# A fused attention and two-stage expert kernel: tails first in the last pair, a branch and the last y moved, first weights loaded behind a transfer

## What is computed

```python
scores = q @ k.T / 8
scores = where(scores >= max(scores) - tau, scores, -1e9)
attn = softmax(scores);  x = (attn @ v)         # heads side by side: 2304 x 512
logits = normed(x) @ normed(expert_emb).T / moe_tau
e = argmax(logits);  gate = softmax(logits)[e]
x = gate * (relu(x @ w1[e]) @ w2[e])            # w1: 512 x 1024, w2: 1024 x 512
h = x @ w_in;  g = max(h, 0) + alpha * min(h, 0)
out = g @ w_out                                 # w_in: 512 x 2048, w_out: 2048 x 512
```

## Time and profile before

| | us |
|---|---|
| median of 3 runs | 1055.79 (1053.36 to 1055.9) |
| the profiled execution | 1049.71 |
| its span, first to last instruction | 1048.0 |
| PE busy in the span | 1018.3 (97%) |
| granted TensorE clock, mean | 0.991 |
| PE busy in 30 to 40 us | 6.82 of 10 |
| PE busy in 60 to 120 us | 59.75 of 60 |
| PE busy in 345 to 375 us | 22.28 of 30 |
| PE busy in 375 to 623 us | 248.00 of 248 |
| PE busy in 623 to 640 us | 14.32 of 17 |
| DVE, ACT, POOL busy in the span | 528.6, 391.0, 336.3 |

### The profile page before, as it was taken

How to read it: one execution, slowest core, us unless ns; L and a number is a source line. 1 busy time by engine, 2 the same in 40 slices (tenths; PEclk the granted TensorE clock), 3 DMA queues, 4 the chain that set the end, 5 groups by cost and what they waited for, 6 DMA issues and landing times.

```text
span 1048.0 us, 19527 instructions
## 1 busy us (share of the span) xinstructions
PE 1018.3 (97%) x6559; PEld 893.6 (85%) x6560; DVE 528.6 (50%) x1203; ACT 391.0 (37%) x814; POOL 336.3 (32%) x443
## 2 busy tenths in 40 slices
PE   8899999999999699999999999999999999999997
PEld 7788898898898578888888878999999899999996
DVE  5778887987987312222221326644444444444442
ACT  5677676776776032222222323221111121111211
POOL 2233334312113596799776361010010010100101
PEclk9999999999999799999999999999999999999999
DMA  5765767767562655465535245000000000000000
GB/s 157 174 140 121 196 168 190 173 161 216 122 143 87 218 191 187 136 199 196 204 127 198 99 164 169 31 25 9 29 31 31 1 30 30 30 0 0 31 1 30
DMA packets 103502, 116.36 MB, mean 111 GB/s; under 512 B 70268, under 2 KB 70300, under 8 KB 102916
## 3 DMA queue, kind: packets, MB, share of 16 engines
q1 hardware_dynamic: 88228, 87.51, 30.2%
q10 hardware_dynamic: 11056, 13.69, 4.1%
q0 software_dynamic: 4144, 14.20, 3.8%
HBM read 68.53 MB, written 18.82 MB: 83 GB/s over the span
## 4 chain that ended last, share of the span: by engine, by line
PE 85%; DMA 4%; DVE 4%; SPq 4%; issue 1%; ACT 1%; POOL 0%; ACTq 0%; POOLq 0%; DVEq 0%
PE bank L682 75%; PE bank L685 9%; DMA k_st<-k_both 3%; SPq L435 1%; SPq L446 1%; DVE probs L1301 1%; DVE neg_max L1293 1%; DVE q_lo L1318 0%; DMA y_sorted<-x_sorted 0%; DMA x_sorted<-X,pos 0%; ACT q_hi L1083 0%; DMA x_row<-x_sorted 0%; SPq L414 0%; SPq L453 0%; SPq L474 0%
## 5 line engine op out<-in xcount | busy, mean ns | idle before, releaser
L682 PE MATMUL bank<-x_hi,ring 128*128 128x384 f32 x768 | 210.8, 337 | 1.3 <-DVE act L1648 1.3
L682 PE MATMUL bank<-ring,g_hi 128*128 128x512 f32 x576 | 179.1, 392 | 0.0
L1235 ACT ACTIVATE g_hi<-act 128x384 fp32r<-128x384 f32 x96 | 50.4, 525 | 303.3 <-DVE act L1648 300.9
L585 POOL TENSOR_TENSOR ring<-stage,ring 128x2048 fp32r<-128x2048 f32 x32 | 147.1, 4598 | 4.8
L682 PEld LDWEIGHTS bank<-x_hi,ring 128*128 128x128 f32 x768 | 140.3, 188 | 5.0 <-DVE act L1648 1.6
L1645 DVE TENSOR_SCALAR neg<-bank,alpha_col 128x384 f32<-128x384 f32 x96 | 59.2, 617 | 144.0 <-PE bank L682 144.0
L682 PE MATMUL bank<-x_lo,ring 128*128 128x384 f32 x384 | 128.9, 336 | 0.0
L1293 DVE TENSOR_REDUCE neg_max<-bank 128x1 f32<-128x576 f32 x144 | 104.3, 753 | 38.0 <-PE bank L682 37.0
L682 PEld LDWEIGHTS bank<-ring,g_hi 128*128 128x128 f32 x576 | 106.8, 188 | 18.7 <-DVE g_lo L1596 0.3
L1067 ACT ACTIVATE probs<-bank,neg_max 128x576 f32<-128x576 f32 x144 | 103.1, 740 | 48.9 <-DVE neg_max L1293 48.8
L682 PE MATMUL bank<-k_st,q_st 128*128 128x288 f32 (+5 forms) x696 | 114.7, 306 | 3.7 <-DVE probs L1301 3.4
(11 more groups left out here) (183 smaller groups left out, 1416.7 us busy)
## 6 DMA issues: line engine op xcount, KB each, us to landing
stage<-in_moe_w SPq DMA_DIRECT2D x32, 1024.0 KB, 5.5
k_st<-k_both SPq DMA_DIRECT2D x60, 288.0 KB
x_row<-x_sorted ACTq DMA_DIRECT2D x23, 296.0 KB, 2.9
y_sorted<-y_row ACTq DMA_DIRECT2D x21, 256.5 KB, 2.6
q_st<-q_hi SPq DMA_DIRECT2D x30, 160.0 KB
q_st<-q_lo SPq DMA_DIRECT2D x30, 160.0 KB
qraw<-in_q SPq DMA_DIRECT2D x16, 256.0 KB, 3.2
vraw<-in_v SPq DMA_DIRECT2D x16, 256.0 KB, 4.9
```

Of the source, the lines that this page charges most:

```text
L585: nc.gpsimd.tensor_tensor(lo, src, hi.bitcast(F32), ALU.subtract).then_inc(piece_lo, 2)
L682: return nc.tensor.matmul(dst, lhsT, rhs, start=start, stop=stop)
L1235: nc.scalar.activation(g_hi[f % 3][:, :], act2[f % 2][:, :], ACT.Copy).then_inc(g_hi_ready, 1)
```

## The change

Five things. (1) In the last pair the tail unit is processed first, so its rows are stored earlier; X's tiles are numbered anew (tail tiles 12 and 13), group 3 is tiles 13 to 15 and group 4 tiles 16 and 17, and DVE and PE weave these two groups into the last units. SP stores both tail halves; ACT did one of them before. (2) `WARM` goes from 26 to 34, and 7 more such matmuls follow `turn_slot(0)`. (3) On PE a slot is cut in two (`slot_first`, `slot_last`), so that the loop's branch comes between `second_first` and `turn_slot` rather than at the slot's end, the last slot's `slot_last` stands behind the loop, and one more expert number is read in each slot. `EARLY` is one lower. (4) In the last stage the last y is copied and stored inside the first blocks, and the pieces of the second matrix start with one rather than two. (5) Expert 0's first weights are no longer loaded at the start: the first 1 MB follows pair 1's spreads and v, the second follows pair 3's spreads.

```diff
-EARLY = MIN_SLOTS - 2
+EARLY = MIN_SLOTS - 3
-WARM = 26
+WARM, WARM_SPLIT = 34, 7
-ROUTES = ((0, 4), (4, 4), (8, 5), (13, 4), (17, 1))
-TAIL_TILES = (12, 17)
+ROUTES = ((0, 4), (4, 4), (8, 5), (13, 3), (16, 2))
+TAIL_TILES = (12, 13)
+        def unit_at(n, j):
+            return (j + UNITS - 1) % UNITS if n == PAIRS - 1 else j
@@ SP
             load_k(sp, 2, 0)
-            load_pieces(sp, 0, 0)
-            load_pieces(sp, 0, 2)
...
-                    if n in (4, 6, 8, 10):
-                        sp.wait_ge(piece_lo, n - 2)
+                    if n in (2, 4, 6, 8, 10):
+                        if n > 2:
+                            sp.wait_ge(piece_lo, n - 2)
                         load_pieces(sp, *((0, n) if n < PIECES else (1, n - PIECES)))
                     if n:
                         sp.wait_ge(pv_done, UNITS * n)
                     load_v(n + 1, 1 - par)
+                    if n == 0:
+                        load_pieces(sp, 0, 0)
...
-            sp.wait_ge(x_ready, UNITS * PAIRS)
-            store_tail(sp, PAIRS - 1, (0,))
+            sp.wait_ge(x_ready, UNITS * (PAIRS - 1) + 1)
+            store_tail(sp, PAIRS - 1, (0, 1))
@@ PE, behind the last pair
             turn_out(last_pair, UNITS - 2)
+            rank(3)
             turn_out(last_pair, UNITS - 1)
-            rank(3)
             rank(4)
@@ PE, slots
+            def slot(i, more):
+                if not static(i):
+                    slot_last(i - 1, None if static(i, 1) else half_of(i - 2))
+                slot_first(i)
...
-            for_slots(pe, slot)
+            for_slots(pe, slot, load_last)
+            last_slot, e_last, half_last, half_before_last = late
+            slot_last(last_slot, half_before_last)
@@ ACT, last stage
-                    if static(g) and f < PIECES - 2:
-                        late_hi_parts(2 + f, 3 + f)
+                    if static(g) and f < PIECES - 1:
+                        late_hi_parts(f + 1, f + 2)
+                    if static(g) and f == 1:
+                        store_y(last_slot)
...
-            late_hi_parts(0, 2)
-            store_y(last_slot)
+            late_hi_parts(0, 1)
@@ DVE, behind the last pair
             normalise(PAIRS - 1, UNITS - 3)
-            normalise(PAIRS - 1, UNITS - 2)
-            normalise(PAIRS - 1, UNITS - 1)
             for k in range(7):
                 route_step(3, k)
+            normalise(PAIRS - 1, UNITS - 2)
             route_step(3, 10)
             for k in (7, 8, 9):
                 route_step(3, k)
+            normalise(PAIRS - 1, UNITS - 1)
@@ DVE, last stage
-            copy_y(last_slot, LAST_BANK)
...
+                    if static(g) and f == 0:
+                        late_lo_parts(0, 1)
                     low(g, f)
-                    if static(g) and f < PIECES - 2:
-                        late_lo_parts(2 + f, 3 + f)
+                    if static(g) and f == 0:
+                        copy_y(last_slot, LAST_BANK)
+                    if static(g) and 0 < f < PIECES:
+                        late_lo_parts(f, f + 1)
-            late_lo_parts(0, 2)
+            dve.wait_ge(late_hi, 1)
```

More of the change, by code:

```diff
@@ L303, in build, with is_tail, heads_of, short @@
         o_stored = [sem(f"o_stored{i}") for i in range(GT)]
+        def unit_at(n, j):
+            return (j + UNITS - 1) % UNITS if n == PAIRS - 1 else j
+        def is_tail(n, j):
+            return unit_at(n, j) == MAIN
+        def heads_of(n, j):
+            return (0,) if is_tail(n, j) else (0, 1)
+        def short(n, j):
+            return 1 if n == PAIRS - 1 and j else 0
         def tile_no(n, j, h=0):
-            return TILES_PAIR * n + 2 * j + h
+            return TILES_PAIR * n + 2 * j + h - short(n, j)
         def turn_no(n, j, w):
-            return TURNS_PAIR * n + (3 * j + w if j < MAIN else 3 * MAIN + (1 if w else 0))
+            return TURNS_PAIR * n + 3 * j - short(n, j) + (w if not is_tail(n, j) else 1 if w else 0)
+        def last_main(n, j):
+            m, i = before(n, j)
+            return last_main(m, i) if is_tail(m, i) else (m, i)
         def before(n, j):
@@ L339, in group_of, with for_slots @@
             return (m, g) if g >= 0 and m < PAIRS else None
-        def for_slots(eng, body):
+        def for_slots(eng, body, between=None):
             end = eng.value_load(slot_end[0:1, EXPERTS - 1:EXPERTS], min_val=MIN_SLOTS + 1, max_val=SLOTS + 1)
@@ L346, in for_slots @@
             body(1, True)
+            if between:
+                between()
             with eng.Fori(2, EARLY) as i:
@@ L606, in small_steps @@
                 for j in range(UNITS):
-                    for h in heads_of(j):
+                    for h in heads_of(n, j):
                         pool.wait_ge(max_ready, tile_no(n, j, h) + 1)
@@ L728, in scores @@
                 if not (static(n) and j == 0):
-                    last_no = tile_no(n, j - 1, h) if j else (tile_no(n - 1, MAIN) if h == 0 else tile_no(n - 1, MAIN - 1, 1))
+                    last_no = tile_no(*last_main(n, j), 1) if h else tile_no(*before(n, j))
                     pe.wait_ge(probs_ready, last_no + 1)
@@ L736, in scores @@
                     jobs = []
-                    for x in (heads_of(0) if j == MAIN else (h,)):
+                    for x in ((0, 1) if u == MAIN else (h,)):
                         for part in range(2):
@@ L747, in scores @@
                     for i, (x, to, keys) in enumerate(jobs):
-                        last = mm(to, q_st[par][:, x, j * P:(j + 1) * P], keys, i == 0, i == len(jobs) - 1)
+                        last = mm(to, q_st[par][:, x, u * P:(u + 1) * P], keys, i == 0, i == len(jobs) - 1)
                 last.then_inc(scores_ready, 1)
@@ L784, in values @@
                 tail = probsT[buf][:, 2 * MAIN * P:2 * SEQ]
-                if j < MAIN:
+                if not is_tail(n, j):
                     for c in range(CHUNKS):
@@ L843, in pair @@
                         scores(*nxt, 0)
-                    if more and nxt[3] < MAIN:
+                    if more and not is_tail(nxt[0], nxt[3]):
                         scores(*nxt, 1)
@@ L886, in _, with warm_up @@
             turn_out(last_pair, UNITS - 2)
+            rank(3)
             turn_out(last_pair, UNITS - 1)
-            rank(3)
             rank(4)
             pe.wait_ge(piece_lo, PIECES)
-            for _ in range(WARM):
-                mm(bank[:, M_BANK, :], ring[:, 0, 0:P], ring[:, 0, 0:D], True, True)
+            def warm_up(n):
+                for _ in range(n):
+                    mm(bank[:, M_BANK, :], ring[:, 0, 0:P], ring[:, 0, 0:D], True, True)
+            warm_up(WARM)
             H_BANK, HT_BANK, X_BANK, Y_BANK = (0, 1), (2, 3), 4, 5
@@ L942, in second_first, with half_of, slot_first @@
                 second(half_at, range(FC - 2))
-            def slot(i, more):
+            def half_of(i):
+                return expert_of(i)[1]
+            def slot_first(i):
                 e, half_at = expert_of(i)
@@ L955, in slot, with slot_last @@
                     second_first(i - 1, e_before, half_before)
+            def slot_last(i, half_before, more=True):
                 if more:
@@ L1328, in normalise @@
                 got = bank[:, turn_bank(n, j), TURN_AT:TURN_AT + TURNED]
-                if j < MAIN:
-                    at_x = x_tile(n, j) * XC + n % 4 * TURNED
+                if not is_tail(n, j):
+                    at_x = x_tile(n, unit_at(n, j)) * XC + n % 4 * TURNED
                     V.tensor_tensor(X[:, at_x:at_x + TURNED].rearrange("p (h d) -> p h d", h=2),
```

44 lines of the change are left out of this document (21 added, 23 removed).

## The result

| | before | after |
|---|---|---|
| median of the timed runs, us | 1054.57 (1053.03 to 1055.9, 4 runs) | 1040.21 (1037.66 to 1042.18, 4 runs) |
| ratio | | 0.9863, 95% interval 0.9835 to 0.9891 |
| the profiled execution, us | 1049.71 | 1037.66 |
| its span, us | 1048.0 | 1036.0 |

The changed kernel is 1.4% faster: 14.4 us by the medians (interval 11.5 to 17.4), 12.0 us between the two profiled executions. The direction was right, and PE's idle times at 34 us, behind the slots and ahead of the last stage are gone as forecast; the sizes were too small.

The account below looks back on a forecast made before the run. PE was taken to bound the kernel, full almost everywhere, so only its idle time could go. The terms -2.9 + 0.2 - 2.4 - 2.7 = -7.8 us took the median from 1055.79 to 1048.0 us, range 1044.5 to 1052.5.

Parts of the forecast that it names:

- Term A: Start: with the weights behind pair 1's spreads, these land earlier and PE's 34 us stall goes; -2.9 us, bounds 1.3 and 3.0.
- term B: Last pair, routing and first slots: earlier scatters and a full clock in slot 0; -2.4 us, bounds 1.0 and 3.1.
- term C: Slots to last stage: PE's waits of 1.42 us (branch) and 1.27 us (DVE's first act) go; -2.7 us.
- term A2: Pair 3: the second MB of weights behind its spreads costs a little; +0.2 us, bounds 0 and 1.2.
- was 6.1 below the median; the terms don't depend on that: Sum: the terms of the profiled execution, 1049.71 us, carry over unchanged to the median, from 1055.79 to 1048.0 us.
- 3.0 if all of the stall goes: Start: upper bound of the gain from moving the weights, PE's stall at 34 us being 2.98 us.
- they end 1.0 us after the rows have landed: Before slot 0: the extra matmuls end at 359.6, the rows land at 358.6, so PE turns them 1.4 us earlier.
- One more register load in each slot: Rival, slots: the third load uses up PE's lead, 1.01 us in each of 19 slots, 1067.2 us; chance 0.04.
- The spreads did get faster: Denies the rival at the start that spreads are no faster without the weights, 1050.9 us; chance 0.10.
- the 1.42 us was no wait for data: Denies the rival at the last slot that PE really waits for data and the moved branch gains nothing, 1049.4 us; chance 0.08.
- the stall of 34 us did not move: Denies the rival that pair 1 then waits on ACT or DVE, or the second MB costs 1.2, about 1049.8; chance 0.07.
- the clock rose during the extra matmuls: Denies the rival before slot 0 that the clock stays low through the extra matmuls, 1051.4 us in all; chance 0.06.

Follow-up runs that it names:

- last_y_only: Kernel before with change 4 alone (last y copied and stored inside the last stage's first blocks): 1054.81 us, ratio 0.9994.
- tails_warm: Kernel before with changes 1 and 2 alone (tail unit first in last pair, 34 extra matmuls and 7 behind the turn): 1050.04 us, ratio 0.996.
- slots_only: Kernel before with change 3 alone (PE's slot cut in two, 18 matmuls queued ahead of the branch): 1054.21 us, ratio 1.0004.
- before_b: Kernel before, unchanged, profiled a second time: 1055.53 us.
- before_c: Kernel before, unchanged, profiled a third time: 1054.70 us.
- weights_only: Kernel before with change 5 alone (expert 0's first two weight loads behind the spreads of pairs 1 and 3): 1047.64 us, ratio 0.9952.
- one_mb_first: Kernel before with only the second 1 MB weight load moved behind pair 3's spreads, the first left at the start: 1053.50 us, ratio 0.9988.

## Why the prediction was wrong in size

The forecast of 1048.0 us was 7.8 us too high. The kernel before itself came out at 1054.57 and not 1055.79, which is 1.2 of them; the other 6.6 are the difference, 14.4 us and not 7.8. No single step explains them.

**First, the sizes of the terms.** Read against the very profile that they were taken from, they sum to 12.0 us and not 7.8. Term A is 2.2 us short, term B 1.0, term C 0.2, and pairs 2 to 14 took 0.6 us less where term A2 had 0.2 more; that stretch differs by up to 3.6 us from profile to profile, so those 0.8 us are within its scatter.

**Second, the step in the sum** that carries the terms over to the median: the profiled execution "was 6.1 below the median; the terms don't depend on that". They do, and this is the other 2.4 us, the largest single step beside term A's size. The first profile was a lucky one in the places that the change empties: its 1.42 us at the branch is the smallest of seven, its start (44.40) the second shortest of eight with the old weights, its 422.40 from hT_lo to the end the shortest of six with the old code there. An idle time that the change removes is worth its mean over executions. Over all profiles with the old code the three stretches take 45.5, 66.5 and 424.2 us, with the new 39.5, 63.0 and 419.5: 6.0 + 3.5 + 4.7 = 14.2 us, close to the 14.4 of the medians.

**Term A, -2.9 forecast.** Profile against profile 5.1, over all profiles 6.0, timed alone 5.1 and, undone in the changed kernel, 7.9. Two steps were off. The duration of the spreads without weights was taken from pair 2, 11.2 us; it was 9.8 to 10.2 in the four profiles whose chain of waits shows it. And "3.0 if all of the stall goes" was no bound. In the first profile PE ran from 22 to 24 us at a granted clock of 0.50, so it came late to the stall and lost less there. In last_y_only and tails_warm, where that fall did not happen, the stall was 5.57 and 5.34 us. And the clock can fall behind the stall, which the term has at nothing: it did so in the six profiles with 2 MB ahead in which PE stood for 3.2 to 5.6 us, not in the two with 2.98 and 2.46. The same place in last_y_only, timeline and busy times:

```profile
38.41 1.12 PE L685 MATMUL bank<-ident,kraw 128*128 128x128 f32 x4 [5.57 <-DVE q_lo L1319]
```
```profile
36.00:40.00 4.00, 1.59 (x7) 1.47 (x8) 1.60 (x4) 3.06 (x7) 0.19 (x1) 0.54 0.57 97
40.00:50.00 10.00, 10.00 (x78) 9.09 (x77) 8.48 (x21) 6.02 (x15) 3.09 (x10) 0.84 0.23 52
```

The landing of the spreads set the time, 34.8 to 36.8 us in the eight kernels with 2 MB ahead of them; PE's stall was only what was left until then. The landing moved by 5.1 us between the first two profiles: 4.1 of them are faster spreads, and the other 1.0 is the lead at 20 us that the weights can't give, which is luck as far as the runs show. From the landing to pair 2's first spread it took 9.0 to 9.1 us in before, slots_only and the profiles with less than 2 MB ahead that show it, and 9.9 to 10.6 in the six whose clock fell behind the stall. So of the 6.0 us over all profiles some 0.9 go with the clock.

**Term A2, +0.2.** Nothing shows it. The stretch of 160 to 180 us, from which its bound of 1.2 was read, isn't the place of the load. Pairs 2 to 14 take 261.8 to 263.4 us with the second MB behind pair 3, 261.8 to 265.5 without.

**Term B, -2.4 forecast, 3.4 in the profiles, 3.5 over all, 4.2 and 3.8 timed.** The last scatter, counted from pair 15's first spread, is 46.74 - 44.10 = 2.6 us earlier (forecast 2.4): the sum of the routing steps, the two tail units and the tail write on DVE was judged rightly, and that write cost nothing. The step that failed is "they end 1.0 us after the rows have landed". The 34 matmuls took 9.61 us and not 10.6, started 2.5 us and not 2.1 ahead of the last scatter, and scatter and rows took 4.41 + 3.52 us, not 4.04 + 3.35, so they ended 0.88 us before. They were faster because the low clock covered fewer of them: the granted clock was 0.50 from 344 to 347 us, where it had been 0.50 from 350 to 356. The slower landings cost 0.5 instead. Slot 0's clock brought its gain: slot 0 to slot 1 went from 9.65 to 8.37 us.

**Term C, -2.7 forecast, 2.9 in the profiles, 4.7 over all, 6.3 timed.** That the 1.42 us are a branch and no wait for data is shown by the branch's own 3.85 us, by slots_only and by PE's start ahead of hT_lo. What the prediction missed: DVE was not simply busy until 636.40, it stood for the landing of an earlier store of y before it could copy the last one, so that in this profile the branch moved alone would have gained nothing; adding up 1.42 and 1.27 was right only because both edits are there. The row of before that says so, in DVE's timeline:

```profile
633.39 0.15 DVE L1557 COPY y_row<-ssq_slot 128x1 f32 x1 [6.43 <-DMA y_sorted<-x_sorted]
```

The other step is the size, 1.42 us for a wait that takes 1.4 to 3.8. Over the six profiles with the old code behind hT_lo PE stood 2.6 us on average at the branch and 0.8 for the first act, and in three of them (before_b, before_c, weights_only) the clock fell behind the branch's wait, for which the term has nothing. That leaves about 1.3 of the 4.7 us to the clock, an estimate: 4.7 - 2.6 - 0.8.

**Rivals.** One more register load in each slot costs nothing: the slots take 252.5 us in both layouts (252.9 in one profile). The spreads did get faster, the 1.42 us was no wait for data, the stall of 34 us did not move, and the clock rose during the extra matmuls.

**Left open.** Timed, term C gives 6.3 us (3.9 to 8.7) where the marks give 4.7, and the weights undone 7.9 where the marks give 6.0; the interval of the first holds both, and for the second none is on record. Why slots_only gains nothing in the median is not known, as said above. Why PE's clock falls at 20 to 26 us in seven of the fourteen profiles (six of them with the weights first, one without) with PE busy in those 6 us is not known.

## What to carry to other kernels

An idle time is worth what it takes on average, with the low clock that may follow it, not what one profile shows: when the profiled execution is well off the median, take further profiles of the unchanged kernel and compare marks before summing up. Read the gain of an earlier transfer at its landing, not from the idle time of whoever waits for it. Two waits in a row for different causes can hide one another, so a part that does nothing alone may still be half of the gain.

## What the runs showed of the hardware

- A compare-and-branch of PE that goes on into the next slot took 0.07 to 0.08 us, the one that leaves the nested branches 3.30 to 4.37 us in ten profiles and 5.92 to 6.20 in four, with one transfer of 16 KB of instructions during it in the ten and two in the four. With 2.85 us of work queued ahead PE stood 1.42 to 3.77 us; with 18 matmuls (4.2 us) queued it never stood in seven profiles, all of the short kind.
- The clock fell to 0.50 behind waits at the branch of 1.95 us (before_b, granted 0.66 over 630 to 635 us), 3.49 (weights_only, 0.50 over 625 to 630), 3.57 (last_y_only, 0.53 over 630 to 635) and 3.77 (before_c, 0.66 over 630 to 635), and not behind 1.42, 1.63 and 3.58 us (before, tails_warm, one_mb_first).
- Eight SBUF copies (160 to 288 KB each) needed 9.8 to 10.2 us from first issue to last landing, 12.5 with 1 MB of weights (one transfer) issued ahead and 13.7 to 15.5 with 2 MB (two).
- The two stores of a slot's y were issued at 626.90 and 627.53 in slots_only and had landed by 633.27, some 6 us later; the median of the kernel before for these stores is 2.6 and 2.8 us.
